# Weights and V stored by the host in tile order: one contiguous run per partition and load

## The reference

```
mask = q_bucket[:, :, :, None] == k_bucket[:, :, None, :]
scores = np.where(mask, scale * q @ k.T, -1e9)
attn = softmax(scores);  x = attn @ v          # -> (1536, 512)
```

```
logits = x @ phi
slot_input = softmax(logits, over tokens).T @ x         # 32 x 512
for e in range(8): slot_out[e] = relu(slot_input[e] @ w1[e]) @ w2[e]
x = softmax(logits, over slots) @ slot_out
```

```
h = x @ w_in;  out = (h - tanh(h)) @ w_out
```

## Time and profile before

| | |
|---|---|
| median of 3 runs | 470.43 us (470.18 to 470.52) |
| the profiled execution, its own time | 470.56 us |
| its span, first to last instruction | 468.8 us, 9796 instructions |
| PE busy | 452.4 us, 97% |
| DVE, ACT, POOL busy | 340.0, 352.7, 162.1 us |
| mean granted TensorE clock | 0.994 of full speed |
| moved by DMA | 67.38 MB in 32784 packets, mean 144 GB/s |

### The profile page before, as it was taken

One profiled execution on the slowest core, in us unless ns is written; L12 is line 12 of the kernel. 1 busy time (PEld: TensorE's weight loads), 2 busy tenths in 40 slices (PEclk: granted clock), 3 DMA queues, 4 the chain that ended last, 5 costly groups with the idle time before them and its releaser, 6 DMA issues.

```text
span 468.8 us, 9796 instructions
## 1 busy us (share of the span) xinstructions
PE 452.4 (97%) x3531; PEld 362.2 (77%) x3531; DVE 340.0 (73%) x776; ACT 352.7 (75%) x675; POOL 162.1 (35%) x230
## 2 busy tenths in 40 slices
PE   8899999999999999999998999888999999999996
PEld 6689888898887988988997434355788888888885
DVE  2767767767767678677674427439999899979991
ACT  6687888878878879788773118049999999989961
POOL 3152451633606335155000010005554454535430
PEclk9899999999999999999999999999999999999999
DMA  8218428165291562722917999990000200020002
GB/s 295 78 44 268 141 73 310 36 213 196 50 340 38 155 246 48 235 63 71 368 48 272 386 387 386 387 337 0 2 1 0 90 2 1 0 91 1 1 0 91
DMA packets 32784, 67.38 MB, mean 144 GB/s; under 512 B 2656, under 2 KB 4576, under 8 KB 32736
## 3 DMA queue, kind: packets, MB, share of 16 engines
q1 hardware_dynamic: 32512, 66.59, 41.9%
q10 hardware_dynamic: 224, 0.16, 0.1%
HBM read 58.09 MB, written 3.15 MB: 131 GB/s over the span
## 4 chain that ended last, share of the span: by engine, by line
PE 91%; DMA 3%; DVE 3%; ACT 1%; issue 1%; POOL 0%; DVEq 0%; ACTq 0%; POOLq 0%
PE b L944 15%; PE b L929 14%; PE b L918 9%; PE b L1117 9%; PE b L1118 9%; PE b L1119 9%; PE b L919 7%; DMA ring_b<-in_w 3%; PE b L1041 3%; PE b L901 3%; PE b L1104 2%; PE b L958 2%; PE b L1081 2%; PE b L980 2%; PE b L960 1%; PE b L998 1%
## 5 line engine op out<-in xcount | busy, mean ns | idle before, releaser
L692 DVE TENSOR_REDUCE st<-b 128x1 f32<-128x768 f32 x96 | 91.5, 953 | 59.1 <-PE b L919 59.1
L434 POOL TENSOR_TENSOR uu<-uu,sq 128x256 f32<-128x256 f32 x94 | 70.6, 773 | 110.3 <-ACT uu L557 110.3
L477 ACT ACTIVATE probs<-b,st 128x768 f32<-128x768 f32 x96 | 95.0, 989 | 10.7 <-DVE st L695 7.5
L488 ACT ACTIVATE pt<-b 128x512 f32<-128x512 f32 x96 | 56.9, 593 | 37.3 <-PE b L929 37.3
L929 PE MATMUL b<-const,probs 128*128 128x128 f32 x576 | 79.8, 275 | 0.5 <-ACT pt L488 0.5
L918 PE MATMUL b<-qk 96*128 96x384 f32 x192 | 74.6, 389 | 1.9 <-ACT probs L477 1.2
L1117 PE MATMUL b<-woh,gh 128*128 128x512 f32 x192 | 75.1, 391 | 0.0
L1118 PE MATMUL b<-wol,gh 128*128 128x512 f32 x192 | 74.8, 389 | 0.0
L929 PEld LDWEIGHTS b<-const,probs 128*128 128x128 f32 x576 | 67.5, 143 | 6.4 <-issue 0.9
L395 POOL TENSOR_TENSOR qk<-raw,qk 64x256 fp32r<-64x256 f32 x48 | 33.7, 726 | 101.8 <-ACT qk L447 101.8
L919 PE MATMUL b<-qk 128*128 128x384 f32 x192 | 65.8, 343 | 0.0
(11 more groups left out here) (130 smaller groups left out, 779.4 us busy)
## 6 DMA issues: line engine op xcount, KB each, us to landing
ring<-in_w SPq DMA_DIRECT2D x16, 1024.0 KB, 9.3
ring_b<-in_w SPq DMA_DIRECT2D x13, 1024.0 KB, 11.6
raw<-in_k SPq DMA_DIRECT2D x16, 384.0 KB, 3.8
raw<-in_q SPq DMA_DIRECT2D x16, 384.0 KB, 4.2
wo_raw<-in_w_out SPq DMA_DIRECT2D x1, 4096.0 KB, 15.3
win<-in_w_in SPq DMA_DIRECT2D x4, 1024.0 KB, 14.3
ring_x<-in_w SPq DMA_DIRECT2D x3, 1024.0 KB, 9.6
out_tiles<-ost SPq DMA_DIRECT2D x12, 256.0 KB, 2.8
```

The lines of the kernel that those rows point to most:

```text
L434: ins = pool.tensor_tensor(uu[:, r, cols], uu[:, r, cols], sq[:, r, cols], ALU.mult)
L477: act.activation(probs[:, h].rearrange("p (a n) -> p a n", a=2), score[h][:, :].rearrange("p (a n) -> p a n", a=2)[:, :, 0:HALF], ACT.Exp, ...
L488: act.activation(pt[:, n % 2, h, 0:PT_A], ptp[:, 0:PT_A], ACT.Copy).then_inc(pt_a, 1)
L692: dve.tensor_reduce(neg, score[h][:, :].rearrange("p (a n) -> p a n", a=2)[:, :, 0:HALF], AX.XY, ALU.max, negate=True).then_inc(max_done, 1)
```

## The change

The host stores w1, w2, w_in and w_out in other orders, in which the 4 blocks of 512 floats that one partition gets by one load stand side by side. So one load of 1 MiB reads one run of 8192 bytes per partition instead of 4 runs of 2048 bytes. w_out is now loaded by four DMAs of 1 MiB instead of one of 4 MiB. `win` in SBUF gets the shape [128, 4, KT, 512] instead of [128, KT, 2048], so that a load is one run there too, and its two readers index it accordingly. V gets a flat shape in HBM and in the load.

```
-    win = sb("win", [P, KT, F2])
+    win = sb("win", [P, 4, KT, 512])
...
-                sp.dma_start(vn[pair % 2][:, :], v[pair]).then_inc(v_loaded[pair % 2], 16)
+                sp.dma_start(vn[pair % 2].rearrange("p h t d -> p (h t d)"), v[pair]).then_inc(v_loaded[pair % 2], 16)
...
-                    src = w1[4 * r + g].rearrange("(k p) n -> p k n", p=P)[:, :, c * 512:(c + 1) * 512]
+                    src = w1[4 * r + g, c]
...
-                    src = w2[e].rearrange("(k p) n -> p k n", p=P)[:, c * KT:(c + 1) * KT, :]
+                    src = w2[e, c]
...
-                sp.dma_start(slot[s], src).then_inc(ring_loaded[s], 16)
+                sp.dma_start(slot[s].rearrange("p k n -> p (k n)"), src).then_inc(ring_loaded[s], 16)
...
-                sp.dma_start(win[:, :, n * 512:(n + 1) * 512], w_in_r[:, :, n * 512:(n + 1) * 512]).then_inc(win_loaded[n], 16)
+                sp.dma_start(win[:, n].rearrange("p k n -> p (k n)"), w_in[n]).then_inc(win_loaded[n], 16)
...
-            sp.dma_start(wo_raw[:, :, :], w_out_r).then_inc(wo_loaded, 16)
+            for n in range(4):
+                sp.dma_start(wo_raw[:, 4 * n:4 * n + 4].rearrange("p k n -> p (k n)"), w_out[n]).then_inc(wo_loaded, 16)
...
-            act.wait_ge(wo_loaded, 16)
+            act.wait_ge(wo_loaded, 64)
...
-                    ins = pe.matmul(ob[i][:, 0:P], sot[:, kt, :], win[:, kt, i * P:(i + 1) * P],
+                    ins = pe.matmul(ob[i][:, 0:P], sot[:, kt, :], win[:, 0, kt, i * P:(i + 1) * P],
...
-                                    win[:, kt, n * 512:(n + 1) * 512], start=True, stop=True)
+                                    win[:, n, kt, :], start=True, stop=True)
...
-        return np.ascontiguousarray(a.reshape(PAIRS, 2, TILES, P, D).transpose(0, 3, 1, 2, 4))
+        return np.ascontiguousarray(a.reshape(PAIRS, 2, TILES, P, D).transpose(0, 3, 1, 2, 4).reshape(PAIRS, P, 2 * TILES * D))
+
+    def by_columns(a):
+
+        lead = a.shape[:-2]
+        t = a.reshape(lead + (KT, P, a.shape[-1] // 512, 512))
+        return np.ascontiguousarray(np.moveaxis(t, (-2, -3), (-4, -3)).reshape(lead + (a.shape[-1] // 512, P, KT * 512)))
+
+    def by_rows(a, blocks):
+
+        lead = a.shape[:-2]
+        t = a.reshape(lead + (blocks, KT, P, 512))
+        return np.ascontiguousarray(np.swapaxes(t, -3, -2).reshape(lead + (blocks, P, KT * 512)))
```

More of the change, by code:

```diff
@@ L58, in bucket_attention_soft_moe_tanh_ffn @@
 def bucket_attention_soft_moe_tanh_ffn(nc, q, k, v, proj, phi, w1, w2, w_in, w_out, consts, out):
-    w_in_r = w_in.rearrange("(k p) n -> p k n", p=P)
-    w_out_r = w_out.rearrange("(k p) n -> p k n", p=P)
     base = 16512
@@ L1202 @@
     laid = {"q": turned(inputs["q"]), "k": turned(inputs["k"]), "v": by_tile(inputs["v"]), "proj": proj, "phi": phi,
-            "w1": inputs["moe_w1"], "w2": inputs["moe_w2"], "w_in": inputs["moe2_w_in"],
-            "w_out": inputs["moe2_w_out"], "consts": consts}
+            "w1": by_columns(inputs["moe_w1"]), "w2": by_rows(inputs["moe_w2"], 2),
+            "w_in": by_columns(inputs["moe2_w_in"]), "w_out": by_rows(inputs["moe2_w_out"], 4), "consts": consts}
     nc = bacc.Bacc("TRN2", target_bir_lowering=False, num_devices=1)
```

## The result

The changed kernel takes 468.18 us, median of 5 runs (467.84 to 468.36), against 470.52 (470.18 to 471.67) of the kernel before on the same chip. The ratio is 0.9946, with a 95% interval of 0.9930 to 0.9961: 2.5 us faster (1.8 to 3.3). Forecast were 467.8 and 2.7 us. The profiled execution took 467.84, its span 466.0, which is 2.8 less than before; both of these executions issue piece 18 at the same time (263.55 and 263.57).

What follows compares the result with a forecast made beforehand. The prediction took PE's waits for the DMA stream of expert pieces as the bound. Its terms, -2.7 us for expert pieces and 0 for the rest, took the median 470.43 to 467.7; it forecast 467.8 us, range 467.1 to 470.4.

Steps and rivals of the forecast that it cites:

- What bounds the kernel: In the mixture of experts, PE waits 4 times for the DMA stream, before pieces 28 to 31, 2.4 us in all.
- V, w_out, win: nothing: Loads of V and w_out and the shape of `win` in SBUF were each to change the time by 0.
- The price of a long packet: Expert and w_in loads: an 8192-byte packet was to take 306.5 ns, saving 0.26 us per load.
- The line through two sizes: Packet times at 2048 and 3072 bytes gave 11.3 ns independent of size plus 36.9 ns per 1024 bytes.
- T: Time of one 1 MiB load of an expert piece or w_in, forecast at 2.45 us in place of 2.72.
- partly faster: Rival: the weight stream has a ceiling of 401 GB/s, piece 31 lands 1.9 us sooner, 468.5 us; chance 0.15.
- no change: Rival: a rate for bytes, in HBM or on the way to SBUF, holds the stream, 470.4 us; chance 0.14.
- slower: Rival: long packets cost more per byte in the weight stream, 471.5 us and more; chance 0.10.
- The sum at piece 31: Savings of the 20 loads up to the last expert piece, up to 5.2 us at its landing.
- second step: Fails if the rate rises but a gap opens behind SP's waits, or VectorE or ScalarE waits where the load stood.
- The cap: PE's own pace of 1.99 to 2.02 us per piece, pieces 28 to 31, limits the gain to 2.7 us.
- Behind the cap: After piece 31 all shifts as one; w_in's first part lands at 303.3, before PE wants it at 306.85.

Runs made afterwards that it cites:

- half27: Kernel before, all runs of 2048 bytes, but only the first half of pieces 27 to 31 loaded; ratio 0.9954 to the kernel before.
- no_early: Kernel before, but pieces 12 to 15 not loaded and the first expert layer reading pieces 4 and 5 instead; ratio 0.9995 to the kernel before.
- run_1024: Changed kernel, but pieces of w1 and w2 stored as 8 blocks of 1024 bytes per partition; ratio 1.0143 to the kernel before.
- run_4096: Changed kernel, but pieces of w1 and w2 stored as 2 blocks of 4096 bytes per partition; ratio 0.9979 to the kernel before.
- all_but_w2: Changed kernel, but w2 read in runs of 2048 bytes as in the kernel before; ratio 1.002 to the kernel before.
- kwa4: Changed kernel with 4 instead of 8 idle transposes ahead of each of pieces 27 to 31; ratio 0.9951 to the kernel before.

## Why the prediction was right, step by step

*What bounds the kernel.* Right, and shown: taking the wait away with less data (`half27`) gives the same time as the change.

*V, w_out, win: nothing.* Within what can be measured, right: w2 alone gives 0.9945, everything but w2 gives nothing. V's packets are in the count of 17200, which came out exactly.

*The price of a long packet.* The line through two sizes held in all: the loads land 3.01, 2.71, 2.56 and 2.48 us apart with runs of 1024, 2048, 4096 and 8192 bytes. An engine moves 64, 32, 16 and 8 packets in a load. From 64 to 32 the load saves 0.30 us, from 32 to 16 0.15, from 16 to 8 some 0.08: 9 to 10 ns for each packet less, where the line had 11.3. T was mis-sized by little: 2.48 measured, 2.45 forecast. The rivals "partly faster" (a ceiling at 401) and "no change" fell with 424 GB/s, and "slower" fell with it too. The Trainium skill's 3 cycles in 67, "DMA: Bandwidth & Descriptors", section "Why small descriptors are slow", gave an estimate of 3.4% less time for the step from 2048 to 8192 bytes; the loads land 2.48 us apart instead of 2.71, 8% less time. Here the measurement decides.

*The sum at piece 31.* This is the step that was off, though the cap hid it. "The 20 loads up to piece 31 would then save up to 5.2 us at its landing, if none of the waits of SP opens a gap", and for piece 18: "no gap". There was one, and by the prediction's own sign its second step failed. Piece 31 landed only 3.1 us sooner, and the last part of w_in at 312.8 instead of 316.8, where the forecast had 309 and 315.

I compared piece 18's first data (265.5) with the landing of piece 17, and a load lands when the last of the 16 engines is done. Before the change 15 of them had finished piece 17 by 266.24 to 266.63 and one, behind since a fetch of q8 at 257.08, at 268.02. The 268.2 that I took was this one engine. After the change the 15 are done between 264.95 and 265.20, ahead of piece 18's data, and the window at 264 us shows the pause. `no_early` shows that nothing saved ahead of piece 18's issue reaches the end. So 14 loads count, those from piece 18 on: 14 x (2.71 - 2.48) = 3.2 us, 3.1 measured. That the two agree so well is in part chance, since the stream also loses time around piece 22, whose wait (`l1_done` 2) the prediction didn't weigh. A stream that gets slower never meets the wait, so there all 20 count: by its pace `run_1024` should lose 20 x (3.01 - 2.71) = 6.0 us, and it shows 6.7 (5.6 to 7.8).

*The cap.* Right in place and size: 2.7 us by PE's own pace, 2.68 us in the trace, 2.5 (1.8 to 3.3) in the times. The reserve was not what the forecast said: a landing at 302.9 against a start at 303.36, 0.45 us instead of 2.5. So the time came out right partly by luck: the 5.2 us of the sum were 3.1, and the cap needed 2.7. With a T only a little longer, the change would have given less, as `run_4096` does.

*Behind the cap.* Right: the first part of w_in landed at 305.4 and not at 303.3, but still ahead of PE's start on it at 306.87, and everything up to the end moved by the same 2.7 us.

What stays open: whether what the one trace of `all_but_w2` shows, engines out of step and a fetch on a late one, is also why its times come out at no gain or a trace slower (1.0001 to 1.0039) rather than the same; and what brings on the second fall of the clock.

## What to carry to other kernels

A load's layout in HBM pays only where a stream of loads is the bound, and then only from the last point on at which the stream has to wait for something else: find the last such issue and count the loads behind it, not all loads in the busy stretch. Whether a wait leaves a gap is told by the engine that is free first, and a landing tells of the one that is free last: here they lay 1.8 us apart. The value of a faster stream ends where the consumer's own pace begins, so read that pace from a place without waits before adding up what the stream could save. Packet durations at two sizes, taken from stretches with one size each, were enough to forecast three other sizes within 3% (3.08, 2.54 and 2.45 us against 3.01, 2.56 and 2.48).

## What the runs showed of the hardware

A DMA packet from HBM to SBUF costs 9 to 10 ns that do not depend on its size: 348, 387, 409 and 424 GB/s on 16 engines with packets of 1024, 2048, 4096 and 8192 bytes, read in windows of 4 us.

A load of 1 MiB lands with the last of its 16 engines. An instruction fetch of 16384 bytes keeps one engine for 1.0 to 1.1 us. Before the change, beside the one at 257.08, one engine fell 1.4 us behind the other 15 (piece 14: 258.18 to 258.51, and 259.88), and it was still so far behind at piece 18.

Without idle transposes PE fell to 1.2 GHz (granted clock 0.50) and was still below full speed when dense work began (0.61); 4 transposes per piece were enough to keep it at 1.00 in all windows from 296 to 320 us of one trace (`kwa4`), and at a mean of 0.996 in all 6 executions of it.
